# Attention of a fused kernel: TensorE's kinds of work grouped over two pairs of units, and keys loaded ahead of values

## The reference

```python
batch, n_heads, seq, head_dim = (2, 8, 768, 64)      # q, k, v, float32
n_global, n_local = (8, 96)
scores = scale * q @ k.T
keep = is_global | is_local                          # key < n_global, or 0 <= row - key < n_local
bias = -slopes * dist
a = softmax(where(keep, scores + bias, -1e9))        # exp, divided by (sum + 1e-9)
x = (a @ v)                                          # to [1536 tokens, 512]
h = x @ w_in1;  x = (h * sigmoid(h)) @ w_out1        # 512 -> 2048 -> 512
h = x @ w_in2;  y = (h * clip(h + 3, 0, 6) / 6) @ w_out2
```

## Time and profile before

| | us |
|---|---|
| median of 3 runs | 596.89 (596.42 to 597.41) |
| the profiled execution's own time | 596.89 |
| its span | 595.1 |
| TensorE busy | 586.8 (99%) |
| VectorE busy | 365.7 (61%) |
| ScalarE busy | 336.1 (56%) |
| GpSimd busy | 267.5 (45%) |

### The profile page before, as it was taken

How to read it: one execution, slowest core, us unless ns; L and a number is a source line. 1 busy time by engine, 2 the same in 40 slices (tenths; PEclk the granted TensorE clock), 3 DMA queues, 4 the chain that set the end, 5 groups by cost and what they waited for, 6 DMA issues and landing times.

```text
span 595.1 us, 9691 instructions
## 1 busy us (share of the span) xinstructions
PE 586.8 (99%) x3477; PEld 523.7 (88%) x3477; DVE 365.7 (61%) x680; ACT 336.1 (56%) x661; POOL 267.5 (45%) x279
## 2 busy tenths in 40 slices
PE   8999899999999999999999999999999999999998
PEld 5777688999999999999999999888888988899996
DVE  6777677768555768557544685475558665554331
ACT  5988785544444756555544675444547655555441
POOL 4665776559433334377333244394332343331110
DMA  8435331222222122122222132112221262111002
GB/s 352 152 128 203 121 121 39 106 72 62 81 72 72 36 70 72 72 70 73 72 71 72 36 105 72 60 48 72 70 72 35 72 204 74 48 65 37 1 0 106
DMA packets 14595, 50.05 MB, mean 84 GB/s; under 512 B 1618, under 2 KB 1874, under 8 KB 14546
## 3 DMA queue, kind: packets, MB, share of 16 engines
q1 hardware_dynamic: 14258, 48.63, 23.8%
q10 hardware_dynamic: 288, 0.79, 0.4%
HBM read 46.27 MB, written 3.15 MB: 83 GB/s over the span
## 4 chain that ended last, share of the span: by engine, by line
PE 92%; DMA 4%; DVE 2%; issue 1%; SPq 0%; ACT 0%; POOL 0%; DVEq 0%
PE ps L1043 39%; PE ps L1130 23%; PE ps L1121 14%; PE ps L1122 7%; PE ps L981 3%; DMA q_raw<-in_qT 3%; PE ps L1015 3%; PE ps L991 3%; DVE g_lo L696 1%; DMA k_raw<-in_kT 1%; PE ps L1000 1%; DVE g_f L553 1%; DVE wi_lo L526 0%; ACT g_hi L901 0%; DVE negs L565 0%
## 5 line engine op out<-in xcount | busy, mean ns | idle before, releaser
L382 POOL TENSOR_TENSOR wo_lo<-wo_raw,wo_hi 128x1024 fp32r<-128x1024 f32 x32 | 77.0, 2407 | 261.1 <-ACT wo_hi L830 255.9
L1043 PE MATMUL ps<-x_hi,wi_hi 128*128 128x384 f32 x448 | 151.2, 337 | 0.7 <-DVE c_sb L543 0.3
L1043 PE MATMUL ps<-x_hi,wi_lo 128*128 128x384 f32 x448 | 150.0, 335 | 0.0
L1043 PE MATMUL ps<-x_lo,wi_hi 128*128 128x384 f32 x448 | 150.0, 335 | 0.0
L543 DVE TENSOR_TENSOR c_sb<-ps,p_c 128x384 f32<-128x384 f32 x64 | 35.6, 557 | 159.6 <-PE ps L1043 159.4
L810 ACT ACTIVATE p_c<-ps 128x384 f32<-128x384 f32 x64 | 31.5, 492 | 128.9 <-PE ps L1043 128.5
L1043 PEld LDWEIGHTS ps<-x_hi,wi_hi 128*128 128x128 f32 x448 | 84.1, 188 | 4.8 <-issue 1.2
L1043 PEld LDWEIGHTS ps<-x_hi,wi_lo 128*128 128x128 f32 x448 | 84.1, 188 | 0.7
L1043 PEld LDWEIGHTS ps<-x_lo,wi_hi 128*128 128x128 f32 x448 | 84.1, 188 | 0.0
L1130 PE MATMUL ps<-wo_hi,g_lo 128*128 128x512 f32 (+1 forms) x194 | 76.3, 393 | 0.0
L1130 PE MATMUL ps<-wo_lo,g_hi 128*128 128x512 f32 (+1 forms) x194 | 76.3, 393 | 0.0
(11 more groups left out here) (104 smaller groups left out, 1082.9 us busy)
## 6 DMA issues: line engine op xcount, KB each, us to landing
wi_raw<-in_w_in SPq DMA_DIRECT2D x32, 512.0 KB, 3.4
wo_raw<-in_w_out SPq DMA_DIRECT2D x32, 512.0 KB, 3.4
v_raw<-in_v SPq DMA_DIRECT2D x8, 704.0 KB, 4.2
k_raw<-in_kT SPq DMA_DIRECT2D x8, 464.0 KB, 4.9
out_y<-y_out SPq DMA_DIRECT2D x11, 256.0 KB, 4.1
q_raw<-in_qT SPq DMA_DIRECT2D x6, 384.0 KB, 5.4
q_raw<-in_qT ACTq DMA_DIRECT2D x2, 384.0 KB, 4.1
out_y<-y_out SPq DMA_DIRECT2D x2, 128.0 KB, 1.9
```

The costliest lines, as they stand in the source:

```text
L382: nc.gpsimd.tensor_tensor(wo_lo[:, s % 2, :], wo_raw[:, s % 2, :], wo_hi[:, s % 2, :], ALU.subtract).then_inc(wo_lo_ok, 1)
L1043: mm = nc.tensor.matmul(p_bank(bank), w[:, s % 2, at], x[:, b, k, :], start=fresh and k == 0 and i == 0, stop=k == 1 and i == 2, skip_grou ...
```

## The change

- **TensorE.** From round 4 on, two rounds are one stage m (`NM` = 12): scores of both, turns of one pair of units' probabilities, values twice, turns of the other pair, then all four units' inverses at once.
- **First tiles.** Their scores are 128 columns wide.
- **VectorE, ScalarE, GpSimd.** Their queues follow: `x_scaled` and `copy_inverses` handle a stage (512 columns), `spread` comes in twos, the last two `x_sum` of the third kind move behind the last spreads.
- **SP.** The values of a head pair are queued behind the keys and queries of the next one.
- **The beginning.** The dummy work is 5 and 4 fp32 products on a block that VectorE sets to 1 first; the mask's global part is computed on 2 x 32 columns and `m_base` is built in place.

```diff
@@ sync, banded
                 for it in range(2, NPAIR):
                     sp.wait_ge(s_done, HALF * (it - 1))
                     load_qk(sp, it)
-                    sp.wait_ge(pv_done, HALF * (it - 1))
-                    load_v(sp, it)
+                    if it > 2:
+                        sp.wait_ge(pv_done, HALF * (it - 2))
+                        load_v(sp, it - 1)
+                sp.wait_ge(pv_done, HALF * (NPAIR - 2))
+                load_v(sp, NPAIR - 1)
@@ gpsimd, banded
+                    if r == 3:
+                        spread(1)
+                    elif r % 2 == 0 and r >= 4:
+                        spread(r - 2)
+                        spread(r - 1)
                     total(r)
...
+                    if r == 1:
+                        spread(0)
...
-                    if r and len(work) < 2:
-                        spread(r - 1)
+                spread(NR - 2)
                 spread(NR - 1)
-                for half in range(2):
-                    x_sum(0, 3, half)
+                for n in (2, 3):
+                    for half in range(2):
+                        x_sum(0, n, half)
@@ vector
+            nc.vector.memset(y_out[:, 0, 0:P], 1.0).then_inc(idle_ok, 1)
...
-                link(nc.vector.tensor_tensor(far, rel8, far, ALU.add))
-                nc.vector.scalar_tensor_tensor(m_base[:, :], glb, nums[:, 3:4], far, ALU.add, ALU.max).then_inc(base_ok, 1)
-                dve.wait_ge(base_ok, 1)
+                link(nc.vector.tensor_tensor(m_base[:, :], rel8, far, ALU.add))
+                for at in GLOB_COLS:
+                    nc.vector.scalar_tensor_tensor(m_base[:, at], glb[:, at], nums[:, 3:4], m_base[:, at], ALU.add,
+                                                   ALU.max).then_inc(base_ok, 1)
+                dve.wait_ge(base_ok, 2)
...
-            def x_scaled(r):
-
-                dve.wait_ge(pv_done, r + 1)
-                nc.vector.tensor_tensor(x_pair(r), o_bank(r)[:, 0:2 * P], inverses[:, r % 2, :], ALU.mult).then_inc(x_ok, 1)
+            def x_scaled(m):
+
+                dve.wait_ge(pv_done, 2 * m + 2)
+                nc.vector.tensor_tensor(x_four(m), ps[:, 0:2, 0:2 * P], inverses[:, :, :], ALU.mult).then_inc(x_ok, 1)
...
+                for m in range(2, NM):
+                    negations(2 * m)
+                    inverse(2 * m - 2)
+                    inverse(2 * m - 1)
+                    negations(2 * m + 1)
+                    copy_t(4 * m - 3)
+                    x_scaled(m - 2)
+                    copy_t(4 * m - 1)
@@ scalar, banded
+                for m in range(2, NM):
+                    exps(4 * m)
+                    exps(4 * m + 1)
+                    if m == 2:
+                        copy_inverses(0)
+                    copy_t(4 * m - 4)
+                    exps(4 * m + 2)
+                    exps(4 * m + 3)
+                    copy_t(4 * m - 2)
+                    copy_inverses(m - 1)
+                    if m == 5:
                         wo_high(0)
@@ tensor
                 for _ in range(n):
-                    nc.tensor.transpose(ps[:, 0, 0:P], ident[:, :], ident[:, :])
-
-            busy(8)
+                    nc.tensor.matmul(ps[:, 0, 0:P], y_out[:, 0, 0:P], y_out[:, 0, 0:P], start=True, stop=True)
+
+            busy(5)
...
-            busy(5)
+            busy(4)
+            pe.wait_ge(ident_ok, 2)
...
-                    first = KS * (t - 1) + GLOB if t else 0
+                    first, width = (KS * (t - 1) + GLOB, 256) if t else (0, P)
...
-            def turn_inverses(r):
-                pe.wait_ge(spread_ok, r + 1)
-                at_least(pe, x_ok, r - 1)
+            def turn_inverses(m):
+                pe.wait_ge(spread_ok, 2 * m + 2)
+                at_least(pe, x_ok, m)
...
+                for m in range(2, NM):
+                    scores(2 * m)
+                    scores(2 * m + 1)
+                    if m == 2:
+                        turn_inverses(0)
+                    turn_pair(2 * m - 2)
+                    values(2 * m - 4)
+                    values(2 * m - 3)
+                    turn_pair(2 * m - 1)
+                    turn_inverses(m - 1)
                 pe.wait_ge(neg_done, 2 * (NU - 2))
                 product(0, P1)
-                turn_probs(NU - 4)
-                turn_probs(NU - 3)
-                turn_inverses(NR - 3)
+                turn_pair(NR - 2)
                 values(NR - 4)
+                values(NR - 3)
                 product(0, P2)
...
+                turn_pair(NR - 1)
+                turn_inverses(NM - 1)
                 product(0, P6)
                 values(NR - 2)
-                product(0, P5)
-                product(0, P7)
-                turn_inverses(NR - 1)
-                product(0, P3)
-                product(0, P4)
+                for n in (P5, P7, P3, P4):
+                    product(0, n)
```

More of the change, by code:

```diff
@@ L19 @@
 NR = NU // 2
+NM = NR // 2
 DM, DF = NH * D, 2048
@@ L405, in banded @@
                         bias(2 * r + 3)
-                    total(r)
-                    work = W_WORK.get(r, ()) + X_WORK.get(r, ())
-                    for i, (kind, which, part) in enumerate(work):
-                        if i == 1:
-                            spread(r - 1)
[L411 to L417, removed]
-                        else:
[L419 to L424, removed]
-                    if r and len(work) < 2:
-                        spread(r - 1)
+                    if r == 3:
[3 more added lines that the diff above has]
+                        spread(r - 1)
+                    total(r)
+                    if r == 1:
+                        spread(0)
+                    for kind, which, part in W_WORK.get(r, ()):
+                        if kind == "s":
+                            w_sum(which, part)
+                        elif kind == "h":
+                            w_high(which, part)
+                        else:
+                            w_low(which, part)
+                    for kind, which, half in X_WORK.get(r, ()):
+                        if kind == "s":
+                            x_sum(0, which, half)
+                        elif kind == "h":
+                            x_high(which)
+                        else:
+                            x_low(which)
+                spread(NR - 2)
                 spread(NR - 1)
-                for half in range(2):
-                    x_sum(0, 3, half)
+                for n in (2, 3):
+                    for half in range(2):
+                        x_sum(0, n, half)
             def general():
@@ L587, in banded, with negations @@
                 base()
-                for r in range(NR):
+                def negations(r):
                     u = 2 * r
-                    if r >= 5:
-                        x_scaled(r - 5)
                     if u % NT == 0 and 0 < u < 4 * NT:
@@ L598, in banded @@
                         negated(k, 1)
[L599 to L605, removed]
+                negations(0)
+                negations(1)
+                inverse(0)
+                copy_t(1)
+                negations(2)
+                inverse(1)
+                negations(3)
+                copy_t(3)
+                for m in range(2, NM):
[6 more added lines that the diff above has]
+                    copy_t(4 * m - 1)
                 inverse(NR - 2)
+                inverse(NR - 1)
                 copy_t(NU - 3)
-                inverse(NR - 1)
-                x_scaled(NR - 4)
+                x_scaled(NM - 2)
                 x_low(0, B22)
@@ L832, in banded @@
             def banded():
-                act.wait_ge(base_ok, 1)
+                act.wait_ge(base_ok, 2)
                 nc.scalar.activation(m_bias[:, 1, :], m_base[:, :], ACT.Copy, scale=slope[:, 1:2]).then_inc(bias0_ok, 1)
[L835 to L838, removed]
-                    if u >= 10 and u % 2 == 0:
-                        copy_t(u - 4)
-                    if u >= 6 and u % 2 == 0:
-                        copy_inverses(u // 2 - 3)
-                    if u == 21:
+                exps(0)
+                exps(1)
+                copy_t(0)
+                exps(2)
+                exps(3)
+                exps(4)
+                copy_t(2)
+                exps(5)
+                exps(6)
+                exps(7)
+                for m in range(2, NM):
[9 more added lines that the diff above has]
+                    if m == 5:
                         wo_high(0)
@@ L1053, in banded @@
                 turn_probs(1)
-                for r in range(3, NR):
-                    scores(r)
-                    turn_probs(2 * r - 4)
-                    turn_probs(2 * r - 3)
-                    turn_inverses(r - 3)
-                    if r >= 4:
-                        values(r - 4)
+                scores(3)
+                turn_pair(1)
+                for m in range(2, NM):
[8 more added lines that the diff above has]
```

(19 more changed lines are left out.)

56 lines of the change are left out of this document (28 added, 28 removed).

## The result

The changed kernel takes 591.72 us (median of 4 runs, 591.02 to 592.77) against 596.65 us beside it; the ratio is 0.9918, 95% interval 0.9899 to 0.9938. Of the forecast 7.1 us some 5 came. The profiled execution took 591.73 us, its span is 590.0 us, 5.1 less than before.

The account below looks back on a forecast made before the run. TensorE's own queue was taken to bound the kernel. Grouping -3.2, narrow scores -1.3, loads -2.45, scaling waits +0.45, the beginning -0.6 and the tail 0 sum to -7.1 us: 596.89 to 589.8, range 587.0 to 592.8.

Parts of the forecast that it names:

- loads: SP's queue: keys and queries, queued before older values, no longer arrive late for scores; -2.45 us.
- narrow scores: First tile of a head pair computes 128 score columns for 256, six such tiles from stage 3 on; -1.3 us.
- grouping, with the waits for scaling: Two rounds per stage remove one S and one V entry in 9 stages, -3.2 us; waits for VectorE's scaling, +0.45.
- the beginning: Start up to `scores(6)`: new dummy products raise the clock sooner, first exps come earlier; -0.6 us (-1.1 to +0.3).
- the tail: End of attention: one V entry fewer, -0.15, against late GpSimd sums and the long scaling, +0.15; 0.
- behind attention: The 499 us after attention are not touched; what attention gives up arrives there whole.
- What bounds the kernel: Time is saved only by shortening TensorE's own queue or ending one of its waits.
- The reckoning by leftovers: TensorE: group start to start less steps is the entry cost, 0.505 us a round, whatever kind of work came before.
- Rival D: Entries are an artefact of modelled ends; only loads and narrow tiles count: -3.7 us, 593.2; chance 0.04.
- Who must keep up: Other engines fit a 6.31 us stage; `turn_inverses` waits for scaling some 0.15 in stages 5, 8, 11: +0.45 us.
- rival B: At the start, TensorE's idleness takes the clock away, doubling work of 2 us: 2 to 2.5 us more, 592; chance 0.05.
- The slower rival: Per stage, VectorE's `inverse(2m-1)` waits for GpSimd's late total, delaying scaling and `turn_inverses`: +9 us, 599; chance 0.03.

Follow-up runs that it names:

- experiment 1: The kernel before with only the change's load order (keys and queries ahead of the older values): 593.65 us, ratio 0.9947 to before.
- experiment 3: The change with the scores of first tiles 256 columns wide again: 592.80 us.
- experiment 6: The change with VectorE's 512-column scaling split into two of 256, the first as soon as the first round's values are done: 590.47 us.
- experiment 4: The change with nine dummy products on TensorE ahead of the first values of stage 2, where it idled: median 591.34 us.
- experiment 5: The change with ScalarE's copy of the first inverses ahead of the exps of units 8 and 9 in stage 2: 589.31 us.
- experiment 2: The change with the loads' old order: 609.19 us, ratio 1.0210 to the kernel before.
- experiment 8: The kernel before with only the change's dummy products in place of dummy transposes: 596.30 us, ratio 0.9988 to before.
- best2: The change with scaling split, first inverses and unit 4 copied before stage 2's exps, unit 5 before its second negations: 588.77 us, 589.53 in a second set.

## Why the prediction was right in direction and 2 us too good

Term by term, in the profiled executions (us, minus is a gain):

| term | predicted | measured |
|---|---|---|
| loads | -2.45 | -2.42 (experiment 1, the middle) |
| narrow scores | -1.3 | -1.25 (experiment 3, by the groups) |
| grouping, with the waits for scaling | -3.2 + 0.45 = -2.75 | -2.23 |
| the beginning | -0.6, of it 0.22 inverses turned early | +1.28 at `scores(6)`, +0.09 of low clock behind them |
| the tail | 0 | -0.61, of it the 0.22 |
| behind attention | 0 | 0 |
| sum | -7.1 | -5.1 |

*What bounds the kernel* was right: TensorE's queue, and what attention gave up arrived at the end whole.

*The reckoning by leftovers* was right: entering a kind of work costs the same whatever came before, also from values to turns. In experiment 6, where groups of 8 no longer wait, 8 second turns take 0.93 us up to the inverses' turns, as the 8 behind scores did before, from 45.64 to

```profile
46.57 0.38 PE L1000 MATMUL ps<-ident,rinv 128*128 128x128 f32 x2
```

(The recorded sum of a stage gives 6.34 as it is written, with steps of 0.11; with 0.109 it is 6.30. The 6.31 used is 6.66 less the two entries.) Adding the waits for scaling (1.1 us, next paragraph) to the 2.23 us that grouping brought gives 3.3 us for the entries removed, 3.2 were forecast. Rival D falls with it. So does the reading by the drain alone (the Trainium skill, TensorEngine Tiling, Key Properties, with the drain of TensorE: Matmul & The Clock Gate, Part 2), an estimated 1.0 us: entering costs three times as much here, and no run separates a drain from the rest of it.

*Who must keep up* named the right place, `turn_inverses` behind the scaling, and undersized it. I allowed 0.15 us in three stages. The scaling took 0.69 us, as bounded, but it ended 0.1 us behind the narrow turns and TensorE followed another 0.15 later (40.29 to 40.44); the inverses' turns then took 0.56 in place of 0.53. That is 0.05 in each of six stages and 0.27 in the three narrow ones, 1.1 us for 0.45. Splitting it gave 0.39 back.

*The beginning* is the step that failed. First exps at 7.50 us, `values(0)` at 18.48 and 2 us of idle TensorE were all as laid out (7.05 to 8.0; with the 10.7 us of ScalarE, 17.75 to 18.7). What I then called harmless, because ScalarE sets this part, was not: values, turns and inverses stand between that idle stretch and `scores(6)`, on TensorE alone, and they ran at 1.2 GHz. That is rival B, priced at 2 us or more and given 0.05; it cost 1.23 us (experiment 4) and came in three of four runs. Without it `scores(6)` would stand at 21.66, within the forecast's 20.8 to 21.75. The Trainium skill (TensorE: Matmul & The Clock Gate, Part 1) says that idleness takes the clock away, and here it did (0.50 from 19.7 us). I had weighed against it a stretch of 1.40 us that was harmless. A stretch longer than any in the trace should have had an even chance, and the cheap cure (experiment 5) was visible from the same layout. This step's own upper bound of +0.3 was passed by some 0.8 us; the total stayed within the range because the other terms came out near their values.

*The loads* came out at their forecast value, but as part of the kernel their role was misjudged: I treated them as one gain beside the others. I never asked what grouping does under the old order. With scores in pairs, every second head pair's first scores stand 3 us behind the release of the keys, and the price is 17.5 us (experiment 2).

*The tail* was put at nothing and gave 0.61: 0.22 are the two turns of inverses done early, and the rest fits the entries. I counted one entry of values fewer, but one of turns and one of products went too (in the tail before stand four groups of values, three of turns and five of products, and after three, two and four), and the 0.15 set against them for late sums and the long scaling did not show: the second step's first product waits 0.29 us for VectorE after and 0.28 before.

*The slower rival* (C, the ring through GpSimd) did not show: VectorE's reciprocals waited for GpSimd once in stage 2 (0.36 us) and once in the tail (0.23), and never in stages 3 to 11.

## What to carry to other kernels

When work is grouped into longer stages, check each load's lead against the new positions before pricing anything: what was late by 1.5 us can become late by 3 to 5, and a change of order elsewhere is then a condition, not an extra. Count an idle stretch of TensorE of about 2 us as the stretch and, in more than half of the runs here (8 of 12), work at half rate behind it, as soon as anything on TensorE's own queue is on the path, and look first for one small instruction in another queue that would end it. Price kinds of work by leftovers (group start to group start, less the steps), which held to a few hundredths of a microsecond per stage here.

## What was not expected of the hardware

- The clock can fall after the work has resumed: idle from 16.54 to 18.48, full steps until 19.7, then 0.50 until 23.1. It did so also in experiment 8 (resumed 72.18, fell 72.9), but in experiment 2 it fell inside both gaps of 3.1 us. An idle stretch of 1.95 us took the clock in two profiles and not in two others with the same stretch; 1.93 us did, 1.40 did not, 3.1 and 4.9 did.
- The first rise differs as much from run to run. Behind the dummy work, the first matmul at the full step of the 2.4 GHz level starts at 10.7 and 9.4 us with the dummy transposes (two profiles) and between 5.7 and 10.5 with the products (eleven), and `best2` alone has both 6.1 and 10.5. Its two profiles differ by 1.6 us at `scores(6)` (19.86 and 21.45) and by as much in their times, most of the 1.9 us between its fastest and slowest run.
